# A delta-rule layer and two feed-forward layers in one kernel: one item's queries loaded at another place in the queue, residuals subtracted ahead of g's low part, the inverse in ten pieces, two unread products in place of eight

## What is computed

```python
# batch 4, 8 heads, 768 times, head dimension 48
for t in range(S):
    y[:, :, t] = q_t @ state                       # read before the update
    v_old = state^T @ k_t                          # k normalised
    state = state + beta_t * outer(k_t, v_t - v_old)
# y laid out as x: 3072 tokens x 384
h = x @ w_in;  g = piecewise square of h;  x = g @ w_out     # d_ff = 2048
h = x @ w_in2; g = relu(h)**2;             out = g @ w_out2
```

## Time and profile before

| what | value |
|---|---|
| median of three runs | 1020.0 us |
| the profiled execution's own time | 1019.98 us |
| its span, first to last instruction | 1018.3 us |
| TensorE busy | 981.3 us (96%) |
| VectorE busy | 603.0 us (59%) |
| ScalarE busy | 406.8 us (40%) |
| GpSimd busy | 39.7 us (4%) |
| mean granted TensorE clock | 0.986 |

### The profile page before, as it was taken

How to read it: one execution, slowest core, us unless ns; L and a number is a source line. 1 busy time by engine, 2 the same in 40 slices (tenths; PEclk the granted TensorE clock), 3 DMA queues, 4 the chain that set the end, 5 groups by cost and what they waited for, 6 DMA issues and landing times.

```text
span 1018.3 us, 24297 instructions
## 1 busy us (share of the span) xinstructions
PE 981.3 (96%) x10230; PEld 799.1 (78%) x10230; DVE 603.0 (59%) x1479; ACT 406.8 (40%) x700; POOL 39.7 (4%) x54
## 2 busy tenths in 40 slices
PE   7999879999989998999899999999999999999998
PEld 6778668777867786788678888888888888888887
DVE  7679757877868776878554775433333334334332
ACT  5567333343433342443343654333333333333323
POOL 5800000000000000000000000000000000000000
PEclk9999979999999999999899999999999999999999
DMA  8422123012101210120002431001010010000000
GB/s 256 145 85 64 49 59 117 18 29 85 53 17 33 80 53 17 34 59 32 2 2 74 173 106 63 1 1 62 1 34 29 1 63 0 1 32 1 32 1 32
DMA packets 28844, 50.75 MB, mean 50 GB/s; under 512 B 2368, under 2 KB 17728, under 8 KB 28736
## 3 DMA queue, kind: packets, MB, share of 16 engines
q1 hardware_dynamic: 28736, 49.19, 14.9%
HBM read 39.75 MB, written 9.44 MB: 48 GB/s over the span
## 4 chain that ended last, share of the span: by engine, by line
PE 89%; DVE 5%; ACT 3%; issue 2%; DMA 1%; SPq 0%; DVEq 0%; ACTq 0%
PE psum L1281 38%; PE psum L1257 36%; PE psum L1029 3%; PE psum L1114 2%; PE psum L1185 2%; PE psum L1054 1%; PE psum L985 1%; PE psum L1000 1%; PE psum L1147 1%; DVE act_g L1577 1%; PE psum L1152 1%; PE psum L1160 1%; PE psum L1168 1%; DVE tmp L1429 1%; DVE x_inv L1433 1%
## 5 line engine op out<-in xcount | busy, mean ns | idle before, releaser
L1281 PE MATMUL psum<-g_hi,w 128*128 128x512 f32 x1152 | 395.0, 398 | 0.0
L1257 PE MATMUL psum<-x_hi,w 128*128 128x512 f32 x1152 | 390.6, 394 | 0.4 <-DVE x_lo L1565 0.4
L1281 PEld LDWEIGHTS psum<-g_hi,w 128*128 128x128 f32 x1152 | 219.4, 190 | 50.2 <-issue 2.4
L1257 PEld LDWEIGHTS psum<-x_hi,w 128*128 128x128 f32 x1152 | 216.3, 188 | 48.4 <-issue 0.6
L1583 DVE TENSOR_TENSOR g_lo<-act_g,g_hi 128x512 fp32r<-128x512 f32 x192 | 132.5, 690 | 202.3 <-ACT g_hi L864 202.2
L1281 PE MATMUL psum<-g_lo,w 128*128 128x512 f32 x576 | 226.9, 394 | 0.0
L864 ACT ACTIVATE g_hi<-act_g 128x512 fp32r<-128x512 f32 x192 | 121.3, 632 | 259.7 <-PE psum L1281 208.3
L1257 PE MATMUL psum<-x_lo,w 128*128 128x512 f32 x576 | 224.3, 389 | 0.0
L851 ACT ACTIVATE act_g<-act_g,half 128x512 f32<-128x512 f32 x87 | 63.0, 724 | 182.6 <-DVE act_g L1572 182.6
L1577 DVE TENSOR_TENSOR act_g<-act_g 128x512 f32<-128x512 f32 x96 | 66.4, 692 | 112.6 <-ACT act_g L857 112.6
L1281 PEld LDWEIGHTS psum<-g_lo,w 128*128 128x128 f32 x576 | 109.9, 191 | 21.7
(11 more groups left out here) (139 smaller groups left out, 644.3 us busy)
## 6 DMA issues: line engine op xcount, KB each, us to landing
kt_sb<-in_k_t SPq DMA_DIRECT2D x24, 256.0 KB, 4.1
qt_sb<-in_q_t SPq DMA_DIRECT2D x23, 256.0 KB, 3.2
ring<-in_v_s SPq DMA_DIRECT2D x24, 192.0 KB, 2.7
between_layers<-y_out SPq DMA_DIRECT2D x6, 768.0 KB, 3.8
x_sb<-between_layers SPq DMA_DIRECT2D x6, 768.0 KB, 5.5
result<-y_out SPq DMA_DIRECT2D x5, 768.0 KB, 3.9
gram_or_states<-in_k_s SPq DMA_DIRECT2D x15, 192.0 KB, 2.4
wi_st<-in_w_in SPq DMA_DIRECT2D x7, 384.0 KB, 3.8
```

The costliest lines, as they stand in the source:

```text
L1257: ins = pe.matmul(h_ps[n % 2][:, :], w_in_part(layer, f // GW, part)[:, kt, fs], x[:, kt, :], start=(kt == 0 and j == 0), stop=(kt == KT - ...
L1281: ins = pe.matmul(acc[kt][:, :], w_out_part(layer, f // GW, part)[:, f % GW, ds], g[n % 2][:, :], start=(f == 0 and j == 0), stop=(f == NF ...
```

## The change

Five edits to the order of work; what is computed stays the same.

1. `load_qt(EARLY_ITEM)` moves from the loop's round n = 1 (behind `load_v(11)`, the last weights of layer 1 and three `load_kt`) to the place right behind the wait for the four outputs of chunk 0.
2. In VectorE's `first_step`, `residual(k)` stands ahead of `g_low(n)`; `masked` of tiles from 1 on stays behind `new_states`.
3. `PIECES` has ten pieces in place of eleven; `turn_inverse` of chunks 3, 4 and 5 thereby comes at `at` = 13, f = 5. The pieces that differ are those of f = 0 to 4: j = 15 to 17, 18 and 19, 20 to 22, 23 to 25, 26 to 30 (before: 15 and 16, 17 to 19, 20 and 21, 22 to 24, 25 to 27, and 28 to 30 in f = 5).
4. `diagonal(2)` in step 9 of tile 0 moves from the first half of `ahead` to the second, behind `activated(9)`, and `CROWDED` is 10: step 9 takes ScalarE's three passes in place of VectorE's clamp and one pass.
5. Of the unread products ahead of chunk 0's solution the seven of `FILLED` go, one of 384 columns is added behind the one of 512, and `SHORT` is 17.

```diff
-        PIECES = (0, 4, 7, 10, 12, 15, 17, 20, 22, 25, 28, BLK - 1)
+        PIECES = (0, 4, 7, 10, 12, 15, 18, 20, 23, 26, BLK - 1)
...
-        SHORT = 10
-        FILLED = (22, 23, 24, 25, 26, 28, 30)
+        SHORT = 17
...
-        CROWDED = 9
+        CROWDED = 10
...
             sp.wait_ge(y_done, B)
+            load_qt(EARLY_ITEM)
             for k in range(NB):
                 load_v(k + RING)
...
-                load_qt(B * n + B - 1)
+                if n > 1:
+                    load_qt(B * n + B - 1)
...
-            for j in FILLED:
-                pe.wait_ge(inv_chain, inv_count(j))
-                keep_busy(3 * P, spare_ps)
             pe.wait_ge(inv_chain, CH)
             keep_busy(4 * P, spare_ps)
+            keep_busy(3 * P, spare_ps)
...
-                if at == 0 and half_of == (t > 0):
+                if at == 0 and half_of:
                     diagonal(n)
...
                     x_low(0, t + 1)
+                k = residual_at(t, f)
+                if k is not None:
+                    residual(k)
                 g_low(n)
                 m = change_at(t, f)
                 if m is not None and m >= B:
                     new_states(m)
-                k = residual_at(t, f)
-                if k is not None:
-                    residual(k)
-                    if t and products_at(t, f) is not None:
-                        masked(products_at(t, f))
+                if k is not None and t and products_at(t, f) is not None:
+                    masked(products_at(t, f))
```

## The result

The changed kernel took 993.7 us in the median (four runs, 991.3 to 997.3), against 1020.1 for the kernel before: a ratio of 0.9746, with a 95% interval of 0.9705 to 0.9787. A second set of its runs gave 992.9 (ratio 0.9721, 0.9706 to 0.9736). One of its six runs was in a slow state, 1204.8 us at a mean clock of 0.756, and counts in that median (992.7 without it) but not in the ratio. Forecast were 990.0, with 985.5 to 1000 as the range. The profiled execution took 991.5 and has a span of 989.7, 28.6 less than before; it is one of the quicker ones.

What follows compares the result with a forecast made beforehand. TensorE was taken to bound the kernel, each stop paid twice, as idle time and slow products behind it. 9.1 + 15.2 + 2.5 + 3.2 = 30.0 us off 1019.98 gave 990.0 us, range 985.5 to 1000.

Steps and rivals of the forecast that it cites:

- Queries: Load of item 7's queries, issued earlier: TensorE's wait for it goes whole, 9.1 us saved, between 6.3 and 9.5.
- Turned inverse one step sooner: Transpose moved ahead of step f = 6 in tiles 2 to 4: three waits go, 15.2 us saved, ends 12 to 15.5.
- The replay: VectorE's order in tile 4 worked through: residual ends near 485.7, TensorE's first product at 486.0, slack 0.3 us.
- what is next late: In tiles 2 to 4, the residual of row block 4n, with 0.3 us of slack in tile 4.
- Residual ahead of g's low part: VectorE's g_low delayed about 0.6 us against over 8 us of slack before second_product: costs nothing.
- rival D: g_low behind the residual becomes what second_product waits for: 45 us lost against 30 gained, 1035 us; chance 0.02.
- step 9 of tile 0: Residual starts 1.93 us sooner, the 3.7 us wait shrinks to 1.8; sum 2.5 us saved, ends 1.2 and 3.2.
- The clock behind that wait: Step 9 of tile 0: whether the clock falls is open; held, it gives back 1.2 us; half taken, 0.6.
- Unread products: Ahead of chunk 0's first solution: TensorE there at 37.5 in place of 40.8; 3.2 us saved, ends 1.7 and 4.1.
- Rival B: Clock low through chunk 0's chain, 41 to 57 us: up to 12.3 us more, 1002 us; chance 0.05.

Runs made afterwards that it cites:

- two single edits: Changed kernel with eleven pieces again, 12.5 us slower than its second set; kernel before with ten pieces and nothing else, 13.8 us faster than before.
- eleven pieces: Changed kernel with the eleven pieces again, so that the transpose stands in f = 6: 1005.4 us.
- queries late: Changed kernel with the queries of item 7 loaded at the old place: 1001.5 us.
- none unread: Changed kernel without the seventeen small and two large unread products ahead of the first solution: 999.7 us.
- step 9 as before: Changed kernel with VectorE's clamp in step 9 of tile 0 and the diagonal's transpose ahead of the activation again: 993.0 us.
- residual put back: Changed kernel with the residual behind g's low part again, all else kept: 993.8 us.
- eight unread: Changed kernel with the eight unread products and ten small ones of the kernel before: 994.0 us.
- the five and the eight traces: Traces of the kernels run: five with eight unread products, eight with two; the layer's first product starts on average at 58.31 and 57.55 us.

## Why the prediction was right, and where it was off

The range held the time, and the waits went as forecast. The forecast was some 3 us too low (990.0 against 992.9 and 993.7).

- **Queries: right.** 9.1 us forecast, 9.3 in the traces, 8.7 to 9.6 in the medians. The first 9.3 are 6.3 of idle time and 2.9 of slow products, as the sum had them. The wait was built into the order of the queue, with no other cover behind it; L1030 takes 1.09 us at the full clock, where 1.14 was worked out from the ratio.
- **Turned inverse one step sooner: right in mechanism, 1 us too high in size.** 15.2 forecast, 14.5 in the traces, 12.5 and 13.8 in the medians of the two single edits. The replay said that the residual would be ready 0.3 us before TensorE asks for it:

```profile
459.44 2.17 DVE L1441 STREAM_TRANSPOSE xc<-x_inv 128x1024 f32<-128x1024 f32 x1
...
462.08 0.54 DVE L1457 TENSOR_TENSOR ring<-ring,psum 128x384 f32<-128x384 f32 x1
...
465.12 0.68 DVE L1571 TENSOR_SCALAR act_g<-psum 128x512 f32<-128x512 f32 x1
...
462.79 0.88 PE L1115 MATMUL psum<-ring,xc 32*32 32x48 f32 x64
...
466.99 0.57 PE L1186 MATMUL psum<-gram_or_states 32*48 32x48 f32 x32 [1.03 <-ACT gram_or_states L769]
...
465.84 0.72 ACT L852 ACTIVATE act_g<-act_g,half 128x512 f32<-128x512 f32 x1 [3.02 <-DVE act_g L1571]
466.47 0.47 ACT L769 ACTIVATE gram_or_states<-psum 128x384 f32<-128x384 f32 x1
```

  The residual (462.08, 0.54) ends 0.2 us before L1115 at 462.79, with no wait: that step held. The one that missed is "what is next late". VectorE is behind, so its clamp of f = 6 comes at 465.12, ScalarE's square pass waits for it, and ScalarE's copy of the solved rows stands behind that pass, though TensorE had them ready from 463.6. `change_by_rows` waits 1.0 us for it. The prediction asked who waits for VectorE, not who waits for ScalarE when it waits for VectorE. This wait is more than the whole gap: tile 3's slow products, counted as tile 2's, cost 1.6 us where 1.5 were taken, and 9.6 + 5.7 - 1.0 makes 14.3, against the 14.5 measured.
- **Residual ahead of g's low part: costs nothing, as forecast,** and rival D with it: no product waited for g's low part in any list of TensorE's waits. But its gain was put under the wrong heading. Of the 1.9 us won in step 9 (forecast 1.9; in the trace 107.85 - 103.11 - 2.8) some 1.4 are the residual's place and 0.5 the clamp; that the transpose's move brings nothing of its own is argued, as said above. The sum was no luck: the 107.85 less 105.92 of the prediction is the clamp's 0.60 and 1.33 for g's low part and its wait, which the residual no longer stands behind.
- **The clock behind that wait: taken as one half, 0.6.** In the traces with a wait of 1.7 to 2.3 us at this place the clock fell in six (changed, eleven pieces, queries late, none unread, step 9 as before, and the residual alone in the kernel before) and stayed in three (second set, residual put back, eight unread). The 2.3 us wait is on both lists, and so is that of 1.8, so its length doesn't decide. In two traces of the changed kernel it fell once, so one half was a fair price. Other lengths say the same: behind waits of 2.8 to 2.9 us in tiles 2 and 3 the clock fell in six cases of eight, and behind the waits of 1.0 to 1.1 us at `change_by_rows` in one of six.
- **Unread products: the term that was mis-sized.** 3.2 us forecast; 2.8 in the first trace, 0.3 in the second, 0.8 between the averages of the five and the eight traces, and 1.1 in the medians of the undone edit. These lines of the changed kernel answer to the earlier trace rows:

```profile
34.18 0.44 PE L1305 MATMUL psum<-later,eye 128*32 128x32 f32 x8 [0.18 <-issue]
34.66 1.77 PE L1169 MATMUL psum<-later,eye 128*128 128x512 f32 x4
36.93 0.93 PE L1103 MATMUL psum<-ring,xc 32*32 32x48 f32 x64 [0.50 <-DVE xc L1441]
...
40.81 0.45 PE L1079 MATMUL psum<-u_sb,gram_or_states 32*32 32x48 f32 x20 [0.81 <-issue]
```

  The count of columns was nearly right (1.77 us, where 1.58 was worked out). TensorE came to the first solution sooner than 37.5 and waited for the transpose, because it began the small products at 32.59; the forecast had taken its 34.29 from one execution, the latest of all the traces. With eight products it began as early as 31.91, and the first solution came at 38.23: part of the 3.9 us between the two first traces was the luck of the start. Two things took back more: a stop of 0.8 us in the chain that nothing in the profile explains, and, in other executions, the clock. Rival B asked whether real work alone holds the clock, and the prediction held against it that the chain keeps unread products of its own. With none ahead of the chain these did not suffice: the clock stayed low to beyond 51 us. With two it depends on the execution. The Trainium skill (TensorE: Matmul & The Clock Gate, section "Why this matters for your kernels") advises to keep TensorE busy to reach the fast clock. This case agrees in part: the kernel without them, where TensorE stood idle 3.5 us first, is 6.8 us slower. But in that kernel TensorE is recorded as busy without a gap from 37.09 to beyond 51 and the clock read 0.50 all the while; there the trace and the advice part, and the measurement stands.

So of some 3 us between forecast and medians, about 2 are this last term and 1 is ScalarE's copy behind its square pass. The 2 rest on medians that the spread of the runs blurs; the 1 is in the trace.

## What to carry to other kernels

When a stop is removed from an engine's order, replay the engines one after another past the place, and ask for each engine that now waits what stands behind it in its own list: here the gain came back as a copy on ScalarE behind a pass that waited for VectorE, and again when a residual was put ahead of a transpose and a root stood in front of the copies. Work whose result is unread can pay for itself in the clock of what follows: two such products were worth 6.8 us against none, while no gain or loss of eight against two is clear. Judge it by the start of the next large block in several executions, not by its own length. And where an edit is a sum of parts, one part undone and one part alone are cheap to run, and put a gain under the right heading.

## What the runs showed of the hardware

The granted clock reads 1.00 in the trace of the kernel before from its beginning up to 109 us, but the column can't be right in its first part. In the changed kernel it reads 0.50 from 20 to 30 us, and the same sixteen products take 2.08 us there in both, which is also what they take at 141.25 in the earlier trace rows, where the clock is 0.50; at full speed they take 1.09. It is likely, and not shown, that the column reads 1.00 until a trace has its first change of clock on record.

```profile
23.75 2.08 PE L1029 MATMUL psum<-qt_sb,kt_sb 48*128 48x128 f32 x16
```

```profile
23.14 2.08 PE L1030 MATMUL psum<-qt_sb,kt_sb 48*128 48x128 f32 x16
```

The other surprise is how much one and the same order of work differs at its start: the layer's first product stood at 56.3 and 58.8 in two executions of the changed kernel, and TensorE made stops in the first 60 us, of 0.2 to 3.1 us each, in every trace, for which no semaphore, load or engine is on record. Their cause was not looked for by any experiment.
